# Two pairs of heads at once in the first layer of token mixing

## The chip, the cores and the metric

The kernel runs on one core of a Trainium2 chip. The metric is the device time in microseconds of one launch. The core's engines are TensorE (PE in the profile, with its weight loads as PEld), VectorE (DVE), ScalarE (ACT), GpSimd (POOL) and SyncE (SP, which issues the loads and stores). They run side by side and wait for each other through semaphores.

## The reference, cut to what matters

Everything is float32. There are 4 batches, 8 heads, 576 positions and a head width of 64, so `x` below is 4 x 576 x 512.

```
scores = q @ k.T / 8                          # per head, 576 x 576
keep   = scores >= rowmax(scores) - tau
attn   = exp(scores - rowmax) where keep, else 0
attn   = attn / (rowsum(attn) + 1e-9)
x      = attn @ v                             # heads side by side: 4 x 576 x 512

h = relu(x.T @ w_tok1) @ w_tok2               # token mixing: 576 -> 256 -> 576
u = x + h.T
y = u + relu(u @ w_ch1) @ w_ch2               # channel mixing: 512 -> 1536 -> 512

g = relu(y @ w_in)                            # 512 -> 1024
c = 3-tap convolution of g over positions
out = (g * sigmoid(c)) @ w_out                # 1024 -> 512
```

## The kernel before

**Split products.** Behind attention, each operand is split into a part rounded to the format fp32r ("h" in the name: `xh`, `wt1h`, `w1h`) and the rest (`xl`, `wt1l`, `w1l`), and a product is made of three matmuls: high by high, high by low, low by high. POOL makes the parts of `x` (`split_x`, L463), of the token weights (`split_wt`, L511), of the channel weights (`split_w1`, L472) and of the hidden tile (`split_hidden`, L482). A split is two instructions: a rounding copy and a subtraction.

**The attention loop.** The work runs over 16 pairs of heads, of one batch each time. A body `k` (g is the same number; inside the hardware loop over k = 4 to 13 it is a register) has five steps s = 0 to 4, one for each query tile of 128 (the last has 64 rows of both heads together). In body k, TensorE makes the scores two tiles ahead, the transposes of the masked probabilities of pair k, the product with v of pair k-1 (`times_v`, steps 0 and 1), and, for pair k-2, token mixing. The bodies go to k = 17. The chain of one tile is: TensorE's scores to PSUM; VectorE copies them out negated, with the row minimum (`copy_out`, L812); ScalarE takes the exponential (L585); VectorE masks and sums (`mask`, L829); TensorE transposes (L993); ScalarE drains (L597). The scores have one place in PSUM, so the next ones (`score_tails` and `scores`) wait for `max_done`, that is for `copy_out`.

**Each engine's order is written out by hand** in its `body`: TensorE's stands at L1136 and behind, ScalarE's at L685, VectorE's at L869, POOL's at L518, SP's below L395. An engine does its list in order, so a wait holds up all that is behind it.

**Token mixing of pair k-2 in body k.** At s=2 TensorE waits for `x_split` and makes the first layer (`mix_hidden`, L1058): for each of five token tiles (the last of 64 rows) and each of the three products one matmul, with the tile of x as the stationary operand (128 channels of the pair) and 256 weight columns moving, so 15 in all. Result: channels on partitions, 256 hidden units beside each other, in PSUM bank `mixed`. In front of them goes a transpose of the 64-row tail of x (L1068). ScalarE applies the relu (`drain_hidden`, L625) into `h1T`; at s=3 TensorE turns this by two transposes (`turn_hidden`, L1082), then turns the output of attention of pair k-1 (`turn_out`, L1045, and its tail, L1049). ScalarE drains the turned hidden tile to `h1f` (L633) behind its exponentials; POOL rounds it to `h1h` (L441) and subtracts to get `h1l` (L489). At s=4 TensorE turns x of pair k-1 (`turn_x`, L1055), waits for `tok_lo`, and makes the second layer (`mix_out`, L1095, 12 matmuls with 288 moving columns) into the banks `out_t` and `mixed`. ScalarE drains these (`drain_u`, L657) and POOL adds x (`add_u`, L496).

**Weights.** SP loads the token weights and the four parts of `w1` at the start. POOL splits the token weights in body 0 to 1 in three big pieces (L441, L455), as soon as the scores of pair 0 are done, and `w1` in 16 pieces of 384 columns (L448, L479), two in body 1, then one in each body to 15. All of w1 is waited for before the first matmul of channel mixing.

**The end of the loop.** Bodies 16 and 17 have no tiles of their own; between the rest of the mixing, TensorE makes the first four chunks of channel mixing's first layer (`hidden`, L1115): chunk 0 at s=3 and 1 at s=4 of body 16, 2 and 3 at s=2 and s=3 of body 17. They need `u` of batch 0 rounded (ScalarE, L684) and its rest (VectorE, L860). Behind the loop `project` (L1130) and `hidden` take turns; VectorE splits w2 between them.

The waits that the prediction speaks of, in the code:

```
def mix_out(pair, k):
    pe.wait_ge(tok_lo, pair + 1)
...
def split_wt():
    pool.wait_ge(s_done, NT)
...
if n == 0:
    pe.wait_ge(w1_split, PAIRS)
```

## Time and profile before

| | us |
|---|---|
| median of 3 runs | 893.38 (892.24 to 894.54) |
| the profiled execution, whole | 894.54 |
| its span in the trace | 892.7 |
| TensorE busy | 847.3 |
| VectorE busy | 429.5 |
| ScalarE busy | 411.2 |
| POOL busy | 278.4 |

The span is the time between the first and the last instruction of the trace. The profile's page gives each engine's busy time, the granted clock of TensorE in forty slices (in tenths of full speed), and the chain of work that ended last. "Waits" sum up which instruction waited for which. The chain of waits follows the work back from the last instruction, in order of time. The timeline lists single instructions with start and duration; matmuls are pipelined, so the duration of one is longer than the distance to the next. "Windows" gives each engine's busy time and the clock in stretches of time.

### The profile page before, as it was taken

Reading aid. Unit: us, or ns where it says so; the run is one execution under the profiler, and the core shown is the slowest. Engines: PE = TensorE matmul, PEld = TensorE weight load, DVE = VectorE, ACT = ScalarE, POOL = GpSimd, SP = SyncE. Lnnn points to the kernel's source line nnn. Section 1 sums busy time; section 2 is a strip of 40 time slices with the busy share of each in tenths; the row PEclk is TensorE's granted clock in tenths of the full one; section 3 lists DMA queues with packets and bytes.
Section 4 is the critical chain, followed back from the end, with each engine's and each line's share of the span. In section 5 each row is a group of like instructions: output and inputs, shape, how many; then the busy total and the mean of one; then the engine's idle time right before and its main releaser. Section 6 shows DMA issues by size and latency. Waiting matters only on the chain.

```text
span 892.7 us, 14832 instructions
## 1 busy us (share of the span) xinstructions
PE 847.3 (95%) x5544; PEld 665.0 (74%) x5544; DVE 429.5 (48%) x828; ACT 411.2 (46%) x866; POOL 278.4 (31%) x218
## 2 busy tenths in 40 slices
PE   7789989999999999889999999999999999999998
PEld 3456656666666666668888888888899989899996
DVE  5877767777777777271121121121121827437280
ACT  4577777777777777522111111121111737457371
POOL 0333333333333333252020020030075463618180
PEclk9799999999999999999999999999999999999999
DMA  9111111111111111400000000000040000010101
GB/s 270 51 50 47 49 48 48 47 47 47 47 47 47 47 48 16 142 1 1 1 1 0 1 1 1 0 1 1 5 161 25 2 23 26 1 59 0 47 0 59
DMA packets 20906, 33.75 MB, mean 38 GB/s; under 512 B 4416, under 2 KB 11136, under 8 KB 20864
## 3 DMA queue, kind: packets, MB, share of 16 engines
q1 hardware_dynamic: 20864, 33.18, 11.4%
q8 instruction: 28, 0.46, 0.2%
q14 instruction: 14, 0.11, 0.0%
HBM read 28.46 MB, written 4.72 MB: 37 GB/s over the span
## 4 chain that ended last, share of the span: by engine, by line
PE 88%; ACT 4%; issue 3%; DVE 2%; POOL 2%; ACTq 0%; POOLq 0%; DVEq 0%
PE score L1115 17%; PE score L1218 11%; PE score L974 6%; PE out_t L1130 4%; PE turn_y L1130 4%; PE mixed L1130 4%; PE tails L1130 4%; PE out_t L1030 4%; PE mixed L1073 4%; PE out_t L1203 4%; PE mixed L1030 4%; PE score L993 3%; PE turn_y L1203 2%; PE mixed L1203 2%; PE tails L1203 2%
## 5 line engine op out<-in xcount | busy, mean ns | idle before, releaser
L812 DVE TENSOR_SCALAR_CACHE_REDUCE negs<-score,neg_scale 128x576 f32<-128x576 f32 x144 | 112.7, 816 | 93.8 <-PE score L974 63.7
L890 DVE SCALAR_TENSOR_TENSOR h<-score,h 128x512 fp32r<-128x512 f32 (+1 forms) x60 | 38.3, 638 | 241.2 <-ACT h L677 241.2
L677 ACT ACTIVATE h<-score 128x512 fp32r<-128x512 f32 (+1 forms) x60 | 33.3, 555 | 255.3 <-PE score L1115 255.3
L829 DVE SCALAR_TENSOR_TENSOR prob<-negs,thresh,exps 128x576 f32<-128x576 f32 x144 | 140.6, 1009 | 0.3 <-ACT thresh L588 0.3
L585 ACT ACTIVATE exps<-negs,neg_max 128x576 f32<-128x576 f32 x144 | 104.9, 776 | 3.2 <-DVE negs L812 2.8
L1115 PE MATMUL score<-uh,w1h 128*128 128x512 f32 (+1 forms) x240 | 89.1, 371 | 3.2 <-DVE ul L860 3.2
L1115 PE MATMUL score<-uh,w1l 128*128 128x512 f32 (+1 forms) x240 | 89.0, 371 | 0.0
L1115 PE MATMUL score<-ul,w1h 128*128 128x512 f32 (+1 forms) x240 | 88.9, 370 | 0.0
L553 POOL TENSOR_TENSOR zl<-z,zh 128x512 fp32r<-128x512 f32 x32 | 54.8, 1711 | 98.7 <-ACT zh_t L751 98.7
L597 ACT ACTIVATE probT<-score 128x512 f32<-128x512 f32 x64 | 38.3, 598 | 80.2 <-PE turn_y L993 80.2
L974 PE MATMUL score<-qk 64*128 64x512 f32 x256 | 74.5, 659 | 0.0
L993 PEld LDWEIGHTS score<-ident,prob 64*128 64x128 f32 x512 | 41.8, 140 | 42.6 <-issue 42.1
L441 POOL TENSOR_SCALAR h1h<-h1f 128x256 fp32r<-128x256 f32 x16 | 7.4, 464 | 211.4 <-ACT h1f L633 211.4
L504 POOL TENSOR_TENSOR ul<-uy,uh 128x256 fp32r<-128x256 f32 (+6 forms) x7 | 16.7, 2398 | 173.9 <-ACT uh L664 173.9
L930 DVE SCALAR_TENSOR_TENSOR conv<-hpad,cw,conv 128x576 f32<-128x576 f32 x32 | 27.3, 853 | 77.5 <-ACT conv L764 77.5
L1218 PE MATMUL score<-yl,wih 128*128 128x288 f32 x256 | 54.8, 296 | 0.0
L1218 PE MATMUL score<-yh,wih 128*128 128x288 f32 x256 | 54.8, 296 | 0.0
L1218 PE MATMUL score<-yh,wil 128*128 128x288 f32 x256 | 54.8, 296 | 0.0
L1115 PEld LDWEIGHTS score<-uh,w1h 128*128 128x128 f32 x240 | 45.7, 190 | 11.3 <-issue 3.4
L1115 PEld LDWEIGHTS score<-ul,w1h 128*128 128x128 f32 x240 | 45.6, 190 | 7.7
L1115 PEld LDWEIGHTS score<-uh,w1l 128*128 128x128 f32 x240 | 45.6, 190 | 7.5
L940 DVE TENSOR_TENSOR z<-hpad,conv 128x576 f32<-128x576 f32 x32 | 50.5, 1578 | 1.1 <-POOL zl_t L555 1.1
(181 smaller groups left out, 2049.3 us busy)
## 6 DMA issues: line engine op xcount, KB each, us to landing
qk<-in_qk SPq DMA_DIRECT2D x16, 704.0 KB, 4.1
vm<-in_v SPq DMA_DIRECT2D x16, 320.0 KB, 4.3
result<-ostage SPq DMA_DIRECT2D x16, 256.0 KB, 2.1
w1f<-in_moe_w_ch SPq DMA_DIRECT2D x4, 768.0 KB, 10.7
w2f<-in_moe_w_ch SPq DMA_DIRECT2D x4, 768.0 KB, 7.0
wif<-in_moe_w_in SPq DMA_DIRECT2D x1, 2048.0 KB, 7.3
wof<-in_moe_w_out SPq DMA_DIRECT2D x8, 256.0 KB, 2.6
wt2f<-in_moe_w_tok SPq DMA_DIRECT2D x1, 576.0 KB, 10.0
```

What stands on the lines that cost most here:

```text
L553: nc.gpsimd.tensor_tensor(zl[:, t, :], z32[:, t % 2, 0:MAIN], zh[:, t, :].bitcast(F32), ALU.subtract)
L585: nc.scalar.activation(exps[i][:, h, :], negs[:, i, h, :], ACT.Exp, bias=neg_max[:, i, h:h + 1], scale=-1.0).then_inc(exp_done, 1)
L812: nc.vector.tensor_scalar(negs[:, i, h, :], raw_of[h], neg_scale[:, 0:1], None, ALU.mult, ALU.min, accum_out=neg_max[:, i, h:h + 1]).then_ ...
L829: nc.vector.scalar_tensor_tensor(out=prob[:, i, h * S:(h + 1) * S], in0=negs[:, i, h, :], scalar=thresh[:, i, h:h + 1], in1=exps[i][:, h, ...
L940: nc.vector.tensor_tensor(z32[:, t % 2, :], hpad[:, t % 3, 1:S + 1], conv[:, t % 3, :], ALU.mult) \
L974: mm = nc.tensor.matmul(score[:, 2 * h, :], qT[par][rows, t * P:(t + 1) * P], kT[par][rows, 0:MAIN])
L993: mm = nc.tensor.transpose(turn[r][:, to:to + D], prob[rows, i, k_at:k_at + P], ident[rows, rows])
L1030: nc.tensor.matmul(bank[mine, 0:HALF], vm[par][:, kt, mine], probT[par][:, h, kt, c * HALF:(c + 1) * HALF], start=(kt == 0), stop=False, s ...
L1115: mm = nc.tensor.matmul(hidden_banks[n % 4][:, 0:w], wt[:, c, kt, :], x[:, kt, 0:w], start=(kt == 0 and i == 0), stop=(kt == KM - 1 and i ...
L1130: mm = nc.tensor.matmul(sum_banks[mt][:, 0:w], wt[:, c, o:o + P], h3[:, n % RING, part, 0:w], start=(c == 0 and i == 0), stop=(c == KC - 1 ...
L1203: mm = nc.tensor.matmul(bank, z, wt[:, kt, :], start=(kt == 0 and n == 0), stop=(kt == KF - 1 and n == 2))
L1218: mm = nc.tensor.matmul(in_banks[c % 2][:, i, 0:HALF], wt[:, kt, c * P:(c + 1) * P], y[:, kt, i * HALF:(i + 1) * HALF], start=(n == 0), st ...
```

## The change

In the first layer a 128x128 tile of the weights becomes the stationary operand and x of two pairs (256 columns) the moving one. The result has hidden units on partitions, so the transposes of `turn_hidden` fall away, and `h1h`, `h1l`, `h1f`, `xh` and `xl` hold two pairs. ScalarE writes the rounded relu to `h1h` and once more in full to `h1f`; POOL only subtracts. `at.hid` is true for odd k from 3 on: both halves of the first layer (`i` = 0, 1: 128 hidden units each, both pairs k-3 and k-2), at s=2 and s=3. `at.mix` is true for even k from 4 on: the second layer of pair k-4 at s=2 and of pair k-3 at s=4. The bodies go to k = 18. The transpose of the 64-row tail of x goes to s=4, among the transposes of the probabilities. The 64-row weight tile is padded with zeros to 128 rows. `xh` and `xl` lie where the last five of twelve chunks of `w1h` come to lie, so these are split after the loop, and the other seven, of 512 columns, in bodies 1, 3, ..., 13. The token weights are split in seven pieces in bodies 1 and 2, once the scores of pair 1 are done.

```diff
--- before.py
+++ after.py
...
+            def split_x(at):
+                pair = at.g - 1
+                mine = slice((at.k - 1) % 2 * P, (at.k - 1) % 2 * P + P)
                 pool.wait_ge(x_done, pair + 1)
                 pool.wait_ge(short_x, pair + 1)
+                if at.hid:
+                    pool.wait_ge(tok_done, at.g - 1)
                 pool.nop(nofuse=True)
-                copy(xh[:, :, :], x32[:, :, :]).then_inc(xs_hi, 1)
+                copy(xh[:, :, mine], x32[:, :, :]).then_inc(xs_hi, 1)
                 pool.wait_ge(xs_hi, pair + 1)
                 pool.nop(nofuse=True)
-                nc.gpsimd.tensor_tensor(xl[:, :, :], x32[:, :, :], xh[:, :, :].bitcast(F32), ALU.subtract) \
+                nc.gpsimd.tensor_tensor(xl[:, :, mine], x32[:, :, :], xh[:, :, mine].bitcast(F32), ALU.subtract) \
                     .then_inc(x_split, 1)
...
+            def split_w1(c, wait):
+                if wait:
+                    pool.wait_ge(w1_loaded, KM * DMA)
                 pool.nop(nofuse=True)
...
+                hi, lo, f = (w[:, :, :, :].rearrange("p c k n -> p c (k n)") for w in (w1h, w1l, w1f))
+                copy_at(hi[:, c, :], f[:, c, :]).then_inc(chunk_hi, 1)
+                pool.wait_ge(chunk_hi, c + 1)
                 pool.nop(nofuse=True)
-                nc.gpsimd.tensor_tensor(lo[:, g, :], f[:, g, :], hi[:, g, :].bitcast(F32), ALU.subtract) \
+                nc.gpsimd.tensor_tensor(lo[:, c, :], f[:, c, :], hi[:, c, :].bitcast(F32), ALU.subtract) \
                     .then_inc(w1_split, 1)
...
-            def split_hidden(pair):
-                pool.wait_ge(hT_drained, pair + 1)
+            def rest_of_token(at, i):
+                pool.wait_ge(hid_left, at.g - 2 + i)
                 pool.nop(nofuse=True)
-                hi, lo = (h[:, :, :].rearrange("p t n -> p (t n)") for h in (h1h, h1l))
-                copy(hi, h1f[:, :]).then_inc(tok_hi, 1)
-                pool.wait_ge(tok_hi, pair + 1)
-                pool.nop(nofuse=True)
-                nc.gpsimd.tensor_tensor(lo, h1f[:, :], hi.bitcast(F32), ALU.subtract).then_inc(tok_lo, 1)
+                nc.gpsimd.tensor_tensor(h1l[:, i, :], h1f[:, i, :], h1h[:, i, :].bitcast(F32), ALU.subtract) \
+                    .then_inc(tok_lo, 1)
...
-            pool.wait_ge(set_once, 1)
-            def split_wt():
-                pool.wait_ge(s_done, NT)
+            pool.wait_ge(set_once, 2)
+            def split_wt(kts):
+                pool.wait_ge(s_done, 2 * NT)
                 pool.wait_ge(wt_loaded, 3 * DMA)
-                split_weight(wt1h[:, 0:FULL, :], wt1l[:, 0:FULL, :], wt1f[:, 0:FULL, :], wt_split)
-                split_weight(wt1h[0:TAIL, FULL, :], wt1l[0:TAIL, FULL, :], wt1f[0:TAIL, FULL, :], wt_split)
-                split_weight(wt2h[:, :, :], wt2l[:, :, :], wt2f[:, :, :], wt_split)
+                for kt in kts:
+                    split_weight(wt1h[:, kt, :], wt1l[:, kt, :], wt1f[:, kt, :], wt_split)
...
             def body(at):
-                g = at.g
-                if at.k == 1:
-                    split_wt()
+                g, k = at.g, at.k
                 if at.mix:
-                    split_hidden(g - 2)
+                    add_u(g - 4)
+                for i in range(KT if at.hid else 0):
+                    rest_of_token(at, i)
                 if at.pv:
-                    split_x(g - 1)
+                    split_x(at)
                 if at.mix:
-                    add_u(g - 2)
-                if at.k == 1:
-                    split_w1(0)
-                if at.units and at.k:
-                    split_w1(g)
+                    add_u(g - 3)
+                if k == 1:
+                    split_wt(range(NT))
+                if k == 2:
+                    for kt in range(KT):
+                        split_weight(wt2h[:, kt, :], wt2l[:, kt, :], wt2f[:, kt, :], wt_split)
+                if k % 2 == 1 and k < 2 * W1_EARLY:
+                    split_w1(g // 2, k == 1)
             bodies(pool, body)
+            for c in range(W1_EARLY, KC):
+                split_w1(c, False)
...
                     else:
+                        if r == 0 and at.pv:
+                            drain_x_tail(g - 1)
...
-            def drain_hidden(pair):
-                act.wait_ge(tok_done, pair + 1)
-                nc.scalar.activation(h1T[:, :], mixed[:, 0:DT], ACT.Relu).then_inc(relu_done, 1)
-                nc.scalar.activation(uy_pair[:, pair, MAIN:S], mixed[:, DT:DT + TAIL], ACT.Copy) \
-                    .then_inc(xt_tail_drained, 1)
-            def drain_turned(pair, k):
-                act.wait_ge(hT_done, pair + 1)
-                if k < PAIRS - 1:
-                    act.wait_ge(xa_tail_done, pair + 2)
-                nc.scalar.activation(h1f[:, :], mixed[:, 0:DT], ACT.Copy).then_inc(hT_drained, 1)
+            def drain_hidden(at, i):
+                act.wait_ge(tok_done, at.g - 2 + i)
+                nc.scalar.activation(h1h[:, i, :], mixed[:, 0:2 * P], ACT.Relu).then_inc(hid_hi, 1)
+                nc.scalar.activation(h1f[:, i, :], mixed[:, 0:2 * P], ACT.Relu).then_inc(hid_left, 1)
...
@@ -688,8 +694,6 @@
                 for s in range(NT):
                     if s == 2 and at.pv:
                         drain_out(g - 1, k - 1)
-                    if s == 2 and k == PAIRS:
-                        round_first_u(0)
...
@@ -697,24 +701,31 @@
                     ahead = at.unit(s + 2)
                     if ahead:
                         exp_unit(ahead)
-                    if s == 2 and at.mix:
-                        drain_hidden(g - 2)
-                    if s == 2 and k == PAIRS:
-                        round_first_u(1)
-                    if s == 2 and k == PAIRS + 1:
-                        unit(0, 2, 3)
-                    if s == 3:
+                    if s == 2:
                         if at.mix:
-                            drain_turned(g - 2, k - 2)
+                            drain_u(g - 4)
+                        if at.hid:
+                            drain_hidden(at, 0)
                         if at.pv:
                             normalise_short(g - 1, k - 1)
-                        if k >= PAIRS:
+                        if k == PAIRS:
+                            round_first_u(0)
+                            round_first_u(1)
+                        if k == PAIRS + 1:
+                            unit(0, 2, 3)
+                    if s == 3:
+                        if at.hid:
+                            drain_hidden(at, 1)
+                        if PAIRS <= k < PAIRS + 2:
                             unit(0, 3 * (k - PAIRS), 3 * (k - PAIRS) + 1)
                     if s == 4:
                         if at.pv:
+                            act.wait_ge(xt_done, g)
+                            if not at.units:
+                                drain_x_tail(g - 1)
                             drain_x(g - 1)
                         if at.mix:
-                            drain_u(g - 2, k - 2)
+                            drain_u(g - 3)
                         if k == PAIRS:
                             unit(0, 1, 2)
...
+            nc.vector.memset(wt1f[TAIL:P, FULL, :], 0.0).then_inc(set_once, 1)
...
-                    dve.wait_ge(tok_done, pair)
+                    dve.wait_ge(x_split, pair)
+                    dve.wait_ge(xt_done, pair)
...
+                    if at.pv:
+                        pe.wait_ge(short_x, g)
+                        pe.nop(nofuse=True)
+                        turn_x_tail()
...
-                    if k >= 2:
-                        pe.wait_ge(u_drained, 2 * (pair - 1))
+                    if k >= 4 and k % 2 == 0:
+                        pe.wait_ge(u_drained, 2 * (pair - 2))
+                    if k >= 3 and k % 2 == 1:
+                        pe.wait_ge(hid_left, pair - 1)
...
-            def turn_out(pair):
-                pe.wait_ge(out_drained, 2 * (pair + 1))
+            def turn_out(at):
+                if at.mix:
+                    pe.wait_ge(u_drained, 2 * (at.g - 4) + 1)
                 for t in range(FULL):
...
-            def mix_hidden(pair, k):
-                if k == 0:
-                    pe.wait_ge(wt_split, 3)
-                pe.wait_ge(x_split, pair + 1)
-                if k < PAIRS - 1:
-                    pe.wait_ge(out_drained, 2 * (pair + 2))
+            def mix_hidden(at, i):
+                g, k = at.g, at.k
+                if i == 0:
+                    if k == 3:
+                        pe.wait_ge(wt_split, NT + KT)
+                    pe.wait_ge(x_split, g - 1)
+                    if k > PAIRS:
+                        pe.wait_ge(u_drained, 2 * (g - 3))
                 else:
-                    pe.wait_ge(u_drained, 2 * pair)
-                pe.nop(nofuse=True)
-                nc.tensor.transpose(mixed[:, DT:DT + TAIL], x32[0:TAIL, FULL, :], ident[0:TAIL, 0:TAIL])
+                    pe.wait_ge(hid_left, g - 2)
+                    if at.pv:
+                        pe.wait_ge(short_x, g)
                 n = 0
                 for kt in range(NT):
-                    w = width[kt]
-                    for x, wt in ((xh, wt1h), (xh, wt1l), (xl, wt1h)):
-                        mm = nc.tensor.matmul(mixed[:, 0:DT], x[0:w, kt, :], wt[0:w, kt, :],
+                    for wt, x in ((wt1h, xh), (wt1l, xh), (wt1h, xl)):
+                        mm = nc.tensor.matmul(mixed[:, 0:2 * P], wt[:, kt, i * P:(i + 1) * P], x[:, kt, :],
                                               start=(n == 0), stop=(n == 3 * NT - 1))
                         n += 1
                 mm.then_inc(tok_done, 1)
...
-            def turn_hidden(pair):
-                pe.wait_ge(relu_done, pair + 1)
-                pe.wait_ge(xt_tail_drained, pair + 1)
-                for m in range(KT):
-                    mm = nc.tensor.transpose(mixed[:, m * P:(m + 1) * P], h1T[:, m * P:(m + 1) * P], ident[:, :])
-                mm.then_inc(hT_done, 1)
...
-            def mix_out(pair, k):
-                pe.wait_ge(tok_lo, pair + 1)
-                if k < PAIRS - 1:
-                    pe.wait_ge(x_done, pair + 2)
-                    pe.wait_ge(short_x, pair + 2)
+            def mix_out(at, i):
+                g, k = at.g, at.k
+                if i == 0:
+                    pe.wait_ge(tok_lo, g - 2)
+                    if k > PAIRS:
+                        pe.wait_ge(u_drained, 2 * (g - 4))
+                else:
+                    pe.wait_ge(u_drained, 2 * (g - 3))
+                    if at.pv:
+                        pe.wait_ge(x_done, g)
+                        pe.wait_ge(short_x, g)
                 for c, bank in enumerate((out_t, mixed)):
                     n = 0
                     for kt in range(KT):
                         for h, wt in ((h1h, wt2h), (h1h, wt2l), (h1l, wt2h)):
-                            mm = nc.tensor.matmul(bank[:, 0:HALF], h[:, kt, :], wt[:, kt, c * HALF:(c + 1) * HALF],
+                            mm = nc.tensor.matmul(bank[:, 0:HALF], h[:, kt, i * P:(i + 1) * P],
+                                                  wt[:, kt, c * HALF:(c + 1) * HALF],
                                                   start=(n == 0), stop=(n == 3 * KT - 1))
                             n += 1
                     mm.then_inc(u_done, 1)
...
-                    pe.wait_ge(w1_split, PAIRS)
...
+                if m == 0:
+                    pe.wait_ge(w1_split, c + 1)
...
-                    if at.mix and s == 2:
-                        mix_hidden(g - 2, k - 2)
+                    if s == 2:
+                        if at.pv:
+                            turn_out_tail(g - 1)
+                        if at.hid:
+                            mix_hidden(at, 0)
+                        if at.mix:
+                            mix_out(at, 0)
                         if k == PAIRS + 1:
                             hidden(2)
                     if s == 3:
-                        if at.mix:
-                            turn_hidden(g - 2)
                         if at.pv:
-                            turn_out(g - 1)
-                            turn_out_tail(g - 1)
-                        if k >= PAIRS:
+                            turn_out(at)
+                        if at.hid:
+                            mix_hidden(at, 1)
+                        if PAIRS <= k < PAIRS + 2:
                             hidden(3 * (k - PAIRS))
                     if at.pv and s == 4:
+                        if not at.units:
+                            pe.wait_ge(short_x, g)
+                            pe.nop(nofuse=True)
+                            turn_x_tail()
                         turn_x(g - 1, k - 1)
                     if at.mix and s == 4:
-                        mix_out(g - 2, k - 2)
+                        mix_out(at, 1)
                         if k == PAIRS:
                             hidden(1)
```

## Rows read from the trace of the kernel before

**Rows 1.** The page: busy time of the engines, and granted clock in forty slices.
```profile
PE 847.3 (95%) x5544; PEld 665.0 (74%) x5544; DVE 429.5 (48%) x828; ACT 411.2 (46%) x866; POOL 278.4 (31%) x218
...
PEclk9799999999999999999999999999999999999999
```

**Rows 2.** Waits, 0 to 400 us: total us, times, longest.
```profile
PE out_t L1095 <- POOL h1l L489: 18.4, 14, 2.2
```

**Rows 3.** The chain of waits through bodies 7 and 8: start, duration, what.
```profile
160.28 1.06 PE score L974 x4
...
166.81 1.06 PE out_t L1095 x6
...
168.89 1.06 PE score L974 x4
...
173.01 1.06 PE score L974 x4
...
180.34 2.16 PE mixed L1073 x15
...
182.91 1.06 PE score L974 x4
```

**Rows 4.** Timeline, steps 3 and 4 of the same body: start, duration, instruction.
```profile
161.92 0.38 PE L1082 MATMUL mixed<-ident,h1T 128*128 128x128 f32 x2
162.14 0.60 PE L1045 MATMUL out_t<-ident,oT 128*128 128x128 f32 x4
...
164.79 0.66 PE L1055 MATMUL tails<-ident,x 128*128 128x128 f32 x4
...
164.84 0.39 ACT L633 ACTIVATE h1f<-mixed 128x256 f32<-128x256 f32 x1
```

**Rows 5.** Masks and POOL: the masks' line (min/median/max ns), then the timeline.
```profile
L829 DVE SCALAR_TENSOR_TENSOR prob<-negs,thresh,exps x144: 754/817/2893, 13.1 to 362.7; 128x576 f32<-128x576 f32 x144
...
166.20 1.16 DVE L829 SCALAR_TENSOR_TENSOR prob<-negs,thresh,exps 128x576 f32<-128x576 f32 x1
...
172.67 1.54 DVE L829 SCALAR_TENSOR_TENSOR prob<-negs,thresh,exps 128x576 f32<-128x576 f32 x1
...
172.27 1.32 POOL L479 TENSOR_TENSOR w1l<-w1f,w1h  x1 [0.15 <-POOL w1h L448]
```

**Rows 6.** Timeline of body 0: the row sum, and a split on POOL.
```profile
28.72 2.47 DVE L837 TENSOR_SCALAR rowsum_pos<-rowsum 128x9 f32<-128x9 f32 x1
...
22.54 2.73 POOL L455 TENSOR_TENSOR wt1l<-wt1f,wt1h 128x1024 fp32r<-128x1024 f32 x1
```

**Rows 7.** Bodies 0 to 3: timeline, the chain, a window (clock is the third last).
```profile
22.74 1.13 PE L974 MATMUL score<-qk 64*128 64x512 f32 x4
...
50.99 1.08 PE score L974 x4
...
54.23 1.13 PE L974 MATMUL score<-qk 64*128 64x512 f32 x4
...
54.48 2.09 DVE L829 SCALAR_TENSOR_TENSOR prob<-negs,thresh,exps 128x576 f32<-128x576 f32 x1
...
77.85 1.13 PE L974 MATMUL score<-qk 64*128 64x512 f32 x4
...
30.00:32.00 2.00, 0.02 (x2) 0.00 (x0) 2.00 (x4) 0.97 (x4) 1.16 (x1) 0.50 0.01 4
```

**Rows 8.** The end of the loop: chain, then a window (clock third last).
```profile
374.87 0.96 issue
...
383.11 4.58 PE score L1115 x12
...
403.06 0.97 PE out_t L1130 x3
...
414.23 2.72 PE score L1115 x12
...
384.00:388.00 4.00, 4.00 (x15) 3.14 (x15) 2.53 (x2) 0.27 (x1) 3.83 (x2) 0.63 0.01 4
```

More of the change, by code:

```diff
@@ L91, in build @@
     w1f = nc.alloc_sbuf_tensor_at("w1f", [P, KC, KM, P], F32, offset=w1l_at)
-    w1_pieces = [w[:, :, :, :].rearrange("p c k n -> p (c k n)").rearrange("p (g n) -> p g n", g=PAIRS)
-                 for w in (w1h, w1l, w1f)]
+    W1_EARLY = 7
+    x_parts = Region(w1l_at - 2 * size([P, NT, 2 * P]))
+    xh = x_parts.put("xh", [P, NT, 2 * P], F32R)
+    xl = x_parts.put("xl", [P, NT, 2 * P], F32R)
+    assert x_parts.at == w1l_at and w1l_at - 2 * size([P, NT, 2 * P]) >= fixed.at + W1_EARLY * size([P, KM, P])
     w2l_at = ch1.at
@@ L133, in build @@
     x32 = s1.put("x32", [P, NT, P])
-    xh = s1.put("xh", [P, NT, P], F32R)
-    xl = s1.put("xl", [P, NT, P], F32R)
-    h1T = s1.put("h1T", [P, DT])
-    h1f = s1.put("h1f", [P, DT])
+    h1f = s1.put("h1f", [P, KT, 2 * P])
     u_part = s1.put("u_part", [P, S])
-    h1h = s1.put("h1h", [P, KT, P], F32R)
-    h1l = s1.put("h1l", [P, KT, P], F32R)
+    h1h = s1.put("h1h", [P, KT, 2 * P], F32R)
+    h1l = s1.put("h1l", [P, KT, 2 * P], F32R)
     wt1h = s1.put("wt1h", [P, NT, DT], F32R)
@@ L310, in __init__ @@
                 self.pv = 1 <= k <= PAIRS
-                self.mix = k >= 2
+                self.hid = k % 2 == 1 and 3 <= k
+                self.mix = k % 2 == 0 and 4 <= k
             def unit(self, n):
@@ L333, in bodies @@
                     body(Pair(2 * j + par, FIRST + par))
-            for k in range(LAST, PAIRS + 2):
+            for k in range(LAST, PAIRS + 3):
                 body(Pair(k, k))
@@ L357, in build @@
         EARLY = 4
+        SHORT_AT = BANK - P
         block = ctx.enter_context(nc.Block())
@@ L639, in normalise_short @@
                 if k >= 1:
-                    act.wait_ge(tok_done, pair)
+                    act.wait_ge(x_split, pair)
                 for h in range(2):
@@ L648, in drain_x, with drain_u @@
             def drain_x(pair):
-                act.wait_ge(xt_done, pair + 1)
                 nc.scalar.activation(uy_pair[:, pair, 0:MAIN], tails[:, :], ACT.Copy).then_inc(xt_drained, 1)
-            def drain_u(pair, k):
+            def drain_u(pair):
                 for c, bank in enumerate((out_t, mixed)):
                     act.wait_ge(u_done, 2 * pair + c + 1)
-                    if c == 0 and k >= 1:
+                    if c == 0 and not (isinstance(pair, int) and pair == 0):
                         act.wait_ge(u_added, pair)
@@ L977, in scores, with turn_x_tail @@
                 mm.then_inc(s_done, 1)
+            def turn_x_tail():
+                return nc.tensor.transpose(turn[0][:, NT * D:NT * D + TAIL], x32[0:TAIL, FULL, :], ident[0:TAIL, 0:TAIL])
             def turn_probs(at, t):
@@ L1048, in turn_out_tail @@
             def turn_out_tail(pair):
-                nc.tensor.transpose(mixed[:, DT:DT + P], oT[:, MAIN:MAIN + 2 * TAIL], ident[:, :]).then_inc(xa_tail_done, 1)
+                pe.wait_ge(out_drained, 2 * (pair + 1))
+                nc.tensor.transpose(mixed[:, SHORT_AT:BANK], oT[:, MAIN:MAIN + 2 * TAIL], ident[:, :]).then_inc(xa_tail_done, 1)
             def turn_x(pair, k):
```

17 lines of the change are left out of this document (6 added, 11 removed).

## The prediction

> **What bounds the kernel now.** The page came first. TensorE is busy for 95% of the span (VectorE for 48%), and its granted clock is full but for a dip in the second of forty slices, 22 to 45 us [rows 1]. So only two things can pay: less work on TensorE, or less time in which it stands still. The attention loop ends near 400 us of 892.7; nothing that the change touches acts behind it, except where the last five chunks of w1 are split.
>
> The waits of the first 400 us say who keeps TensorE standing: of the waits that stand before a matmul the largest entry is POOL's h1l, 18.4 us in 14 [rows 2]. The chain of waits through one pair shows its place [rows 3]. From scores to scores a pair takes 182.91 - 160.28 = 22.63 us. Each of its five steps begins with its scores: s=3 with s=4 take 8.61 us (to 168.89), s=0 4.12 (to 173.01), s=1 with s=2 9.90. In s=4 the second layer of token mixing stands at the end of a row of engines: ScalarE drains the turned hidden tile at 164.84, behind its exponentials, POOL rounds it and subtracts, and TensorE starts at 166.81, having ended turn_x at 165.45: 1.36 us of nothing [rows 3, 4]. 14 x 1.36 = 19 us, the 18.4 of the waits.
>
> Then what stands right behind, since it is late next. VectorE's copy of the scores, which has to be out before the next ones are written, is a floor: in k=1, with no mixing at all, one step still takes 54.23 - 50.99 = 3.2 us [rows 7]. And VectorE's masks take 0.82 us in the median but 1.16 and more, up to 1.54, while POOL computes [rows 5]: the two of s=4, from 166.20, end near 168.6, when TensorE, late itself, has not begun the scores of 168.89. This is hidden today by the 1.36 us.
>
> **The change part by part.**
>
> *Matmuls of the first layer: nothing.* Each instruction now has a weight tile as stationary and two pairs (256 columns) as moving operand; before it had the x tile and 256 weight columns. Two pairs took 2 x 15 instructions of 256 columns and take 2 x 15 now, each with its own load. 15 of them take 2.16 us [rows 3]; before and behind the last three of 64 rows some 0.1 us is lost each, and those are now padded to 128 rows: -0.2 us a pair.
>
> *Turning the hidden tile: gone.* The two transposes L1082 and their switch lie between 161.92 and 162.14 [rows 4]: -0.22 us a pair. ScalarE has two relus of 128x256 (0.39 each by L633 [rows 4]) in place of relu and copy: nothing. POOL loses the rounding h1h, less than half of the 1.6 us from 165.23 to 166.81 [rows 3, 4]. The x tail's transpose only moves from s=2 to s=4; turn_out_tail moves from s=3 to s=2: nothing.
>
> *The order.* Odd k carries both first layers (s=2, s=3), even k both second layers (s=2, s=4), each of pairs whose hidden tile was ready one k earlier. The 1.36 us wait goes. What comes in its place, in us after the scores of s=3 (160.28):
> Odd k: turned probabilities (L1045 ends them, in 0.44 [rows 4]) and turn_out end near 2.1, 15 matmuls with their switch to 4.2, next scores at 4.6 (now 3.14). The new wait for hid_left is covered: both relus follow the matmuls of s=2, which end 0.5 before, so they are done at 0.3, and TensorE asks at 2.1. In s=4 only turn_x is left, so the copy is the floor: scores 4.6 to 5.65, copy done at 7.2, next scores 7.6. s=3 and s=4 take 7.6 us against 8.61: -1.0. VectorE starts the masks of the next tile at 7.3. POOL, which takes the two subtractions, xh, xl and then a w1 chunk, works until about 12.4, so these masks are long, 2.4 us together as those from 166.20 on [rows 5], and end at 9.7. TensorE has its scores at 8.65 and wants them: +1.0 in s=0 of the even k.
> Even k: s=3 has only turn_out and sits on the floor, 3.14. s=4: scores to 4.2, turning to 5.3, mix_out 1.86 to 7.2, next scores 7.4: -1.2 against 8.61. Masks end at 8.2 even if long, before TensorE's 8.5. ScalarE drains u until 8.95, and times_v asks for it at 8.9: +0.1. mix_out in s=2 is 1.86 where 2.16 and the tail's bubble were: -0.25. s=1 loses its wait for long masks, since POOL has nothing but add_u there: -0.3 in both kinds.
> Sum for odd and even: (-1.0 - 0.2 - 0.3 + 0.1) + (-1.2 + 1.0 - 0.25 - 0.3) = -2.15 us in two pairs, -1.1 a pair. For k=3 to 15 that is 13 x 1.1 = -14.3 us. Bounds: without any long mask on the path -1.65 a pair (-21.5); if two thirds of it are taken back, -0.5 a pair (-6.5). I take -1.1, because the long masks are in the rows of every pair.
> At this place the Trainium skill speaks against the change (SBUF - State Buffer, "Who interferes with whom"): a VectorE instruction with two SBUF inputs waits for a GpSimd instruction that reads SBUF to end, and the other way round. The trace agrees: a sum of 9 numbers took 2.47 us while wt2l ran [rows 6]. By that rule each POOL instruction can add at most its own length, and w1 pieces grow from 384 to 512 columns. What it would make if it decides is rival C.
>
> *Splitting the token weights: later and in small pieces.* Now they are split in k=0. The longest mask of all, 2.89 us [rows 5], stands beside wt1l (from 22.54 on), a row sum of 9 columns takes 2.47 us beside wt2l; TensorE starves, and from 30 us on the clock is at 1.2 GHz, for some ten us [rows 6, 7]. After the change the pool waits for the scores of k=1 and takes 256 or 576 columns at a time. k=0 and k=1 then go by undisturbed steps: from scores at 22.74, s=3 and s=4 3.1 (the floor, without turn_x), s=0 4.1, s=1 5.0, s=2 2.6 (one head to copy), s=3 and s=4 3.3 each, which is 47.2 for the scores of k=2's s=0, now 54.23 [rows 3, 7]: -7.0 us. The splits then fall on k=2, whose first two masks already take long (2.09 us) beside two w1 pieces [rows 7], and on the first step of k=3: +0.7, by half a long pair of masks. Bounds of this part: 0 (the same stall and dip elsewhere) to -10.
>
> *Work that moves to the end.* k=2 mixes nothing. Now k=2 takes 54.23 to 77.85 = 23.6 us; without mixing 5.5 + 5.2 + 2.6 + 3.3 + 3.2 = 19.8: -3.9 us, which must come back. The end now: from the last times_v (374.87) to the first project (403.06) 28.2 us [rows 8]. New, counted from T, the same point: mix_out of pair 12 to T+2.9, turn_out 3.45; then the rounding of u on ScalarE and its rest on VectorE, the same four instructions as now, one place later for ScalarE and with fewer in front of them, and so hidden(0) at T+8.0, as now (383.11, which is 8.24); with a clock dip as now (0.63 [rows 8]), 4.4 us; turn_x and mix_out 13 to 14.7, hidden(1) 17.5, first layer 19.5, hidden(2) 22.2, first layer 24.1, hidden(3) 26.9, mix_out 14 to 28.6, mix_out 15 (waits 0.5 for the drain) 30.9, drained 31.45, project at T+31.5: +3.3 us. Bounds +1 and +8 (5 more of clock, by the ten half-speed us of k=0).
> The five late w1 chunks take POOL about 3 us each, of it 1.32 x 4/3 for the subtraction by the 384-column piece [rows 5], from about T+33; so the one that hidden(7) needs is there at T+36. Now hidden(5) begins 11.2 us behind the first project [rows 8], hidden(7) thus 22 behind, at T+53: nothing. If that cover were gone, 3 us. The added xh/xl wait (tok_done) stands in front of the POOL queue of add_u and w1 only, both with many us of room. SP's queue issues the same loads at the same places. The zeroing of 64x256 is one short instruction before the first scores' copy: nothing, at most 0.3.
>
> **The sum.** -7.0 + 0.7 - 3.9 - 14.3 + 3.3 = -21.2 us. The profiled execution took 894.54 us (span 892.7), which gives 873.3; it was the slowest of the three, 1.2 above the median 893.38, so the forecast is 872.2, rounded 872 us.
>
> **The rivals.**
> *A, the loop keeps the whole gap*: POOL's shorter work frees the masks, -1.65 a pair, 872 - 7 = 865 us. For: POOL loses the rounding and a third of w1. Against: its work in the odd k stays in one piece from 5.4 to 12.4. Chance 0.14.
> *B, the start gives nothing*: the token splits stall k=1 to k=3 as they did k=0, or the clock dips there. 872 + 7 = 879, with a dip at the end as well 883. For: the same engines, and 54.48's mask already took 2.09 us [rows 7]. Against: pieces of 0.7 to 1.4 us, and TensorE has turning and times_v there. Chance 0.2.
> *C, slower*: VectorE becomes the bound. If the masks of s=4 and s=0 take 2.09 us each (as at 54.48) and not 1.2, those of s=4 end 1.8 us later, TensorE waits that in each k, and the copy queued behind them pushes s=1 by some 0.6: +2.4 a pair, 13 x 2.4 = +31, 903 us. It decides from 1.85 us a pair (24 us) on. For: the copies, masks and sums are all on VectorE, and nothing behind them moves without them. Against: VectorE has a quarter of each pair to spare, and a mask as long came up once after k=0 [rows 5, 7]. Chance 0.08.
> *D, the end*: clock at half for ten us more in k=16 to k=18, 877. Chance 0.08.
>
> **How the numbers follow.** The forecast has 0.5, with a range of its own of 866 to 879. With A at 865 and B and D inside, 861 to 885 holds a bit over 0.8; C and part of B's upper end lie outside. About 0.3% (2.7 us) is what can be told from no change. Faster: forecast, A, D and nearly all of B, 0.88; same 0.04 (between B's end and C); slower 0.08.
>
> **What would show it.** The wait of TensorE for h1l is gone, and no wait for hid_left or tok_lo over 0.5 us stands in its place. Odd and even k alternate, near 21.2 and 21.9 us. Scores of k=2 begin near 47 us with a clock of 1.0 throughout; no mask over 2.2 us in the first 50 us. From the last times_v to project 31 to 32 us. It is wrong if masks of about 2 us stand in every pair, if the clock dips again before 60 us, or if the stretch from project on changes its length by over 1 us.

## The result, and the profile after

The changed kernel takes 868.71 us in the median of 4 runs (868.62 to 869.71); the kernel before, run beside it, 893.86. The ratio is 0.9724, with a 95% interval of 0.9707 to 0.9741: faster by 2.8%, or 24.7 us. The forecast was 872 us, with a range of 861 to 885.

The page of the kernel after, the lines that answer to [rows 1]:

```profile
PE 826.0 (95%) x5512; PEld 655.8 (76%) x5512; DVE 420.9 (49%) x829; ACT 411.0 (47%) x866; POOL 263.7 (30%) x202
...
PEclk9999999999999999899999999999999999999999
```

The dip of the clock in the second slice is gone; in the seventeenth one shows, which was shorter before (there the clock was 0.63 from 384 to 388 us [rows 8]). Its waits over the first 400 us, the three in front of TensorE's matmuls that matter, in total us, times, longest (compare [rows 2]):

```profile
PE score L975 <- DVE negs L824: 15.6, 22, 1.5
...
PE score L1010 <- DVE prob L841: 7.7, 8, 1.1
...
PE score L1142 <- DVE ul L873: 6.1, 1, 6.1
```

The 18.4 us for POOL's h1l are gone from the loop. In their place other waits have grown: for VectorE's copies of the scores from 9.8 us to 15.6, for its masks (L841, as L829 before) from 3.1 to 7.7, and one at the end from 3.2 to 6.1. The chain of waits through bodies 7 and 8 (compare [rows 3]; L987 and L989 are the scores, L1099 the first layer, L1120 the second):

```profile
156.00 1.06 PE score L987 x4
...
161.04 0.92 PE score L989 x2
...
162.96 1.79 PE mixed L1099 x15
164.75 0.22 PE score L975 x2
164.97 1.06 PE score L987 x4
...
167.22 1.79 PE mixed L1099 x15
...
169.24 1.08 PE score L987 x4
...
172.04 2.72 DVE prob L841 x4
...
178.00 1.06 PE score L987 x4
...
183.04 0.91 PE score L989 x2
...
186.77 1.06 PE score L987 x4
...
198.22 1.06 PE score L987 x4
```

From scores of s=1 to the next such scores the odd body takes 178.00 - 156.00 = 22.0 us, the even one 198.22 - 178.00 = 20.2 us, together 42.2 where two bodies took 45.3. The lines left out of this chain are TensorE's, the copies of the scores, and ScalarE's exponentials and drains at the end of the even body, behind which TensorE stands for 0.18 us. Its longest wait in these bodies is for the masks from 172.04 on, at the turn from the odd to the even body: 1.11 us. The timeline shows what lies beside them (start, duration, instruction; in brackets how long the engine stood before it):

```profile
172.05 2.07 POOL L472 TENSOR_TENSOR xl<-x,xh 128x640 fp32r<-128x640 f32 x1
...
172.64 2.10 DVE L841 SCALAR_TENSOR_TENSOR prob<-negs,thresh,exps 128x576 f32<-128x576 f32 x1
...
174.89 0.25 PE L1010 MATMUL score<-ident,prob 64*128 64x64 f32 x1 [1.11 <-DVE prob L841]
```

At the start, the first scores of body 2 come at 47.04, not 54.23 [rows 7], and those of body 3 at 65.92, not 77.85:

```profile
47.04 1.13 PE L987 MATMUL score<-qk 64*128 64x512 f32 x4
...
65.92 1.13 PE L987 MATMUL score<-qk 64*128 64x512 f32 x4
```

The end of the loop (compare [rows 8]), the chain of waits and one window, whose third last number is the clock:

```profile
346.94 0.39 issue
...
350.56 2.56 DVE ul L873
353.37 4.88 PE score L1142 x12
...
369.75 0.39 ACT h1h L639
370.55 1.99 POOL h1l L491
372.58 1.06 PE out_t L1120 x6
...
377.33 0.95 PE out_t L1157 x3
...
353.00:357.00 4.00, 3.63 (x9) 2.89 (x10) 2.74 (x3) 0.00 (x0) 0.00 (x0) 0.50 0.00 0
```

Between 346.9 and 353.4 TensorE has nothing but waits for the rest of the first chunk of u, and `hidden(0)` (L1142) then runs mostly at 1.2 GHz. From the last times_v (344.0) to the first project (377.33) it is 33.3 us, 28.2 before. From there to the end both kernels need the same: 867.0 - 377.33 = 489.7 and 892.7 - 403.06 = 489.6.

The account of the two spans, cut by the scores (forecast behind the stroke): to body 2 -7.2 us / -7.0, body 2 -4.7 / -3.9, body 3 to the last times_v -18.9 / -13.6, from there to project +5.1 / +3.3; together -25.7, the difference of the spans, / -21.2.

### The profile page after: what moved, and what is told of

Its sections match the earlier page's. It is cut to its first block, busy times and chain, and to the rows that moved or that the text cites. A ratio compares the mean times of both kernels' runs of the same rounds, so it can differ in the third digit from the quotient of the medians.

```text
span 867.0 us, 14725 instructions
## 1 busy us (share of the span) xinstructions
PE 826.0 (95%) x5512; PEld 655.8 (76%) x5512; DVE 420.9 (49%) x829; ACT 411.0 (47%) x866; POOL 263.7 (30%) x202
## 4 chain that ended last, share of the span: by engine, by line
PE 86%; DVE 5%; ACT 4%; issue 4%; DMA 1%; POOL 0%; DVEq 0%; ACTq 0%; SPq 0%; POOLq 0%
PE score L1142 17%; PE score L1253 12%; PE score L987 5%; PE out_t L1157 4%; PE turn_y L1157 4%; PE mixed L1157 4%; PE tails L1157 4%; PE out_t L1053 4%; PE out_t L1238 4%; PE mixed L1053 4%; PE mixed L1099 3%; PE score L1010 3%; PE turn_y L1238 3%; PE mixed L1238 3%; PE tails L1238 3%
## 5 line engine op out<-in xcount | busy, mean ns | idle before, releaser
L683 ACT ACTIVATE h<-score 128x512 fp32r<-128x512 f32 (+1 forms) x60 | 33.3, 555 | 256.5 <-PE score L1142 256.5
L841 DVE SCALAR_TENSOR_TENSOR prob<-negs,thresh,exps 128x576 f32<-128x576 f32 x144 | 133.7, 960 | 0.3 <-ACT thresh L595 0.3
L1142 PE MATMUL score<-uh,w1h 128*128 128x512 f32 (+1 forms) x240 | 89.2, 372 | 6.1 <-DVE ul L873 6.1
L1142 PE MATMUL score<-ul,w1h 128*128 128x512 f32 (+1 forms) x240 | 89.0, 371 | 0.0
L1142 PE MATMUL score<-uh,w1l 128*128 128x512 f32 (+1 forms) x240 | 89.0, 371 | 0.0
L1010 PEld LDWEIGHTS score<-ident,prob 64*128 64x128 f32 x512 | 41.0, 139 | 45.3 <-issue 45.2
L987 PE MATMUL score<-qk 64*128 64x512 f32 x256 | 72.3, 641 | 0.0
L1142 PEld LDWEIGHTS score<-uh,w1h 128*128 128x128 f32 x240 | 45.8, 191 | 13.9 <-issue 6.3
L499 POOL TENSOR_TENSOR uy<-u_part,uy 128x576 f32 (+1 forms) x16 | 23.5, 1471 | 96.9 <-ACT u_part L663 96.9
L1010 PE MATMUL score<-ident,prob 64*128 64x64 f32 x512 | 44.6, 224 | 7.8 <-DVE prob L841 7.7
L1142 PEld LDWEIGHTS score<-uh,w1l 128*128 128x128 f32 x240 | 45.7, 190 | 7.7
L1142 PEld LDWEIGHTS score<-ul,w1h 128*128 128x128 f32 x240 | 45.7, 190 | 7.6
```

Source lines behind the costliest of these rows:

```text
L841: nc.vector.scalar_tensor_tensor(out=prob[:, i, h * S:(h + 1) * S], in0=negs[:, i, h, :], scalar=thresh[:, i, h:h + 1], in1=exps[i][:, h, ...
L987: mm = nc.tensor.matmul(score[:, 2 * h, :], qT[par][rows, t * P:(t + 1) * P], kT[par][rows, 0:MAIN])
L1010: mm = nc.tensor.transpose(turn[r][:, to:to + D], prob[rows, i, k_at:k_at + P], ident[rows, rows])
L1142: mm = nc.tensor.matmul(hidden_banks[n % 4][:, 0:w], wt[:, c, kt, :], x[:, kt, 0:w], start=(kt == 0 and i == 0), stop=(kt == KM - 1 and i ...
```

## The experiments

Ratios are to the kernel before, run on the same chip in turns, with 95% intervals.

### The token weights later, alone (e1)

```diff
 def split_wt():
-    pool.wait_ge(s_done, NT)
+    pool.wait_ge(s_done, 2 * NT)
-    split_weight(wt1h[:, 0:FULL, :], ...)
+    for kt in range(FULL):
+        split_weight(wt1h[:, kt, :], ...)
...
-    split_weight(wt2h[:, :, :], ...)
+    for kt in range(KT):
+        split_weight(wt2h[:, kt, :], ...)
```

It is called behind `split_x` in body 1.

> The kernel before, with one part of the change alone: the token weights are split in seven pieces of 256 and 576 columns once the scores of pair 1 are done, in body 1, not in three big ones once those of pair 0 are. Theory (the stall of body 0 and the clock's fall behind it are made by these splits and don't come back): scores of body 2 near 49 us in place of 55.3, the clock full throughout the first 50 us, 886 to 888 us in all. Rival (the stall only moves to bodies 1 and 2, or the clock falls there): 892 or more.

890.82 us, ratio 0.9961 (0.9947 to 0.9976): between the two. Scores of body 2 begin at 47.71, so the stall of body 0 is gone and didn't come back in body 1. But in this kernel body 2 mixes already, and its first layer waits 2.50 us for the last piece. The chain of waits of this kernel:

```profile
60.67 1.78 POOL wt2l L455
62.46 0.14 issue
62.59 0.24 PE mixed L1069
62.84 3.65 PE mixed L1074 x15
```

15 matmuls take 3.65 us in place of 2.16: behind the wait the clock is at half for 3.4 us, from 62.9 on. From scores to scores, s=2 of body 2 takes 8.72 us, not 4.70. The seven runs lie between 888.6 and 892.9 us, the shorter ones with the higher mean clock; only one of the longer was traced. The late moment thus pays only where body 2 doesn't mix, as in the change.

### The token weights at the early moment, in small pieces (e8)

```diff
 def split_wt():
     pool.wait_ge(s_done, NT)
-    split_weight(wt1h[:, 0:FULL, :], ...)
+    for kt in range(FULL):
+        split_weight(wt1h[:, kt, :], ...)
...
-    split_weight(wt2h[:, :, :], ...)
+    for kt in range(KT):
+        split_weight(wt2h[:, kt, :], ...)
```

> The kernel before, with the token weights split at the early time of body 0, but in seven small pieces. Theory by size (a long POOL subtraction blocks one mask for its whole length): no mask over 1.6 us, body 1 begins 2 us earlier or more, and with TensorE less idle the clock stays full, 887 to 889. Rival by moment (POOL is busy at body 0 in any case and blocks mask behind mask): the same stall, clock dip near 29 us, 892 to 895.

888.35 us, ratio 0.9938 (0.9923 to 0.9953): the theory by size. Beside pieces of 256 columns the two masks that took 0.94 and 2.89 us now take (its timeline):

```profile
22.18 1.12 DVE L831 SCALAR_TENSOR_TENSOR prob<-negs,thresh,exps 128x576 f32<-128x576 f32 x1
...
22.65 0.91 POOL L441 TENSOR_SCALAR wt1h<-wt1f 128x256 fp32r<-128x256 f32 x1
...
23.23 0.94 DVE L831 SCALAR_TENSOR_TENSOR prob<-negs,thresh,exps 128x576 f32<-128x576 f32 x1
```

The clock stays full until 377 us. One expectation failed, that no mask takes over 1.6 us: one of 1.95 stands beside the second layer's piece of 576 columns, and one of 2.08 (at 49.41) beside `xl`.

```profile
29.51 1.79 POOL L455 TENSOR_TENSOR wt2l<-wt2f,wt2h 128x576 fp32r<-128x576 f32 x1
...
29.97 1.95 DVE L831 SCALAR_TENSOR_TENSOR prob<-negs,thresh,exps 128x576 f32<-128x576 f32 x1
```

The scores of body 2 begin at 49.16, where they began at 54.23 before and begin at 47.04 in the change. So the size of the pieces is the greater part of the start's gain, 5.1 us here and 5.5 in all; the moment is the smaller.

### Distance alone (e2), and with small pieces (e10)

The kernel before, one pair at a time with its transposes, but `mix_out`, `drain_u` and `add_u` for pair k-3, and `h1h` and `h1l` in two buffers each:

```diff
-    h1h = s1.put("h1h", [P, KT, P], F32R)
+    h1h = [s1.put(f"h1h{i}", [P, KT, P], F32R) for i in range(2)]
...
-                    if at.mix and s == 4:
-                        mix_out(g - 2, k - 2)
+                    if at.out and s == 4:
+                        mix_out(g - 3, k - 3)
```

> The kernel before, with one pair at a time as it was, transposes and all, but the second layer of token mixing one body later (pair k-3, hidden tile in two buffers). Theory (the loop's gain is the wait for POOL's h1l, which distance alone removes): bodies of 21.4 us in place of 22.6, 13 of them, some 3 us back at the end, 880 to 884 us. Rival (the gain comes from two pairs at once: no transposes, no ScalarE copy, other matmul forms): bodies of 22.2 or more, 889 or more.

881.81 us, ratio 0.9871 (0.9856 to 0.9886). Bodies 3 to 14 take 21.7 us each, copy to copy, where they took 22.6. The clock's dip at the start is still there. So distance alone is worth 11.5 us, 0.9 us a body.

e10 adds the diff of e8 to this one.

> The kernel before with two parts at once: the second layer one body later, and the token weights in seven small pieces at the early time. What is left to the changed kernel is two pairs at once with weights stationary, no transposes of the hidden tile, the padded tile. If the parts add: 893.8 - 12 - 5.4 = 876.4 us, and the new form of the first layer is worth some 7.5 us (868.7). If the form is worth nothing: 869 to 871.

877.74 us beside 894.69, ratio 0.9811 (0.9796 to 0.9826), which is -16.9 us on 893.8; e2 and e8 by themselves give -11.5 and -5.5, so these parts add. The change has -24.7. The rest, 7.8 us (the two intervals leave 6 to 10), belongs to what e10 lacks: two pairs at once, no transposes, the padded tile, the later moment and the split of w1.

### The last tile at 64 rows again (e3, e9)

```diff
+                    w = width[kt]
...
-                        mm = nc.tensor.matmul(mixed[:, 0:2 * P], wt[:, kt, i * P:(i + 1) * P], x[:, kt, :],
+                        mm = nc.tensor.matmul(mixed[:, 0:2 * P], wt[0:w, kt, i * P:(i + 1) * P], x[0:w, kt, :],
```

> The changed kernel, with the last token tile of the first layer at 64 rows again (its matmuls read half of the rows; the sums are the same). Theory (TensorE loses time at each change between 64 and 128 rows): 15 matmuls of the first layer take 2.0 to 2.2 us in place of 1.79, 16 times, 872 to 874 us. Rival (the height costs nothing, the first layer's steps became shorter for another reason): 1.8 us, 868.7.

882.78 us, ratio 0.9874 (0.9859 to 0.9889): 14 us slower than the change, three times what the theory said. The height costs what was said: in each odd body s=2 and s=3 are 0.39 and 0.37 us longer. The rest is in the chain, TensorE's waits and a window of this kernel in the turn from body 5 to body 6:

```profile
133.80 3.31 DVE prob L841 x4
...
137.86 1.16 PE out_t L1053 x4
...
135.74 0.24 PE L1010 MATMUL score<-ident,prob 64*128 64x64 f32 x1 [0.39 <-DVE prob L841]
...
137.25 0.24 PE L1010 MATMUL score<-ident,prob 64*128 64x64 f32 x1 [1.05 <-DVE prob L841]
...
137.00:141.00 4.00, 3.75 (x22) 2.12 (x24) 3.15 (x10) 2.59 (x5) 1.22 (x1) 0.57 0.00 0
```

Two masks hold the chain for 3.31 us, not 2.72, TensorE stands twice (1.44 us in all, where it stood 1.06 us in the change), and the clock falls for 3.4 us. Of the six turns of the loop four have the fall and take 7.6 to 7.8 us for s=0; two, with the same waits (0.43 and 1.04 us at 181), have none and take 6.1 to 6.2, where the change takes 5.5 to 5.6. To tell height from this, e9 puts the same edit on e7 (below), in which POOL leaves these masks alone.

> The last token tile of the first layer at 64 rows again, this time in the kernel whose POOL leaves the masks alone (x split first, w1 behind the masks; 862.9 us with 128 rows). Theory (of the 14 us that 64 rows cost in the changed kernel some 5.5 are TensorE's changes of height, 0.39 + 0.37 us in each of 7 odd bodies; the rest is that the masks came to lie worse beside POOL's reads, and the clock fell in the wait behind them): no dip in the loop, 867.5 to 869.5 us. Rival (the height itself costs all of it): 875 to 877.

867.16 us against 862.89 with 128 rows: 4.3 us for the height by the medians, 3.6 by the ratios (0.9695 and 0.9655), a little less than said, and no dip in the loop. The chain of e9, 15 matmuls and the scores' first piece behind them, to be compared with 162.96 and 164.75 above:

```profile
162.11 1.97 PE mixed L1104 x15
164.08 0.42 PE score L979 x2
```

1.97 for 1.79 and 0.42 for 0.22: 0.19 us on each of two changes of height.

### POOL's order in odd bodies (e4, e7)

```diff
-                for i in range(KT if at.hid else 0):
-                    rest_of_token(at, i)
+                if at.hid:
+                    rest_of_token(at, 0)
                 if at.pv:
                     split_x(at)
+                if at.hid:
+                    rest_of_token(at, 1)
```

> The changed kernel, with one POOL order changed in odd bodies: the split of x goes ahead of the second subtraction of the hidden tile, so that it begins some 1.5 us earlier and ends near where the masks of the next pair's first tile begin. Theory (that mask takes 2.10 us because it waits for POOL's 2.07 us subtraction of x, and TensorE waits for the mask): the mask takes 1.3 us or less, odd bodies get 0.5 to 1.0 us shorter, 7 of them, 862 to 865 us. Rival (POOL then has the w1 chunk beside the same mask, which blocks it as long): no change, 868 to 869.

867.77 us, ratio 0.971 (0.9696 to 0.9723): the rival, near enough; the turn takes 5.3 us and not 5.5. The split of x is over before the masks, but the w1 chunk now lies beside them (timeline of e4):

```profile
171.84 1.56 POOL L448 TENSOR_TENSOR w1h<-w1f,ones 128x512 f32 x1
...
172.43 1.58 DVE L843 SCALAR_TENSOR_TENSOR prob<-negs,thresh,exps 128x576 f32<-128x576 f32 x1
```

e7 takes this chunk away as well:

```diff
+                if k % 2 == 0 and 4 <= k <= 2 * W1_EARLY:
+                    pool.wait_ge(mask_done, TILES * g + 4)
+                    split_w1(g // 2 - 1, False)
...
-                if k % 2 == 1 and k < 2 * W1_EARLY:
-                    split_w1(g // 2, k == 1)
```

(chunk 0 stays in body 1.)

> The changed kernel with the split of x ahead of the second subtraction, and the w1 chunk of an odd body taken in the next even body, behind the masks of its second tile. Theory (in odd bodies TensorE waits for two masks, and they for whatever POOL reads then; with nothing beside them they take 0.82 us): the masks at the turn from odd to even bodies take 0.8 to 1.1 us, odd bodies 21.2 us or less in place of 22.2, 861 to 864 us. Rival (VectorE's own queue is the floor there): 867 to 868.

862.89 us, ratio 0.9655 (0.9642 to 0.9668). By its chain of waits the odd body takes 174.72 - 153.73 = 21.0 us, 22.0 in the change:

```profile
153.73 1.06 PE score L991 x4
...
174.72 1.06 PE score L991 x4
```

The two masks of the turn (timeline of e7):

```profile
169.69 1.03 DVE L845 SCALAR_TENSOR_TENSOR prob<-negs,thresh,exps 128x576 f32<-128x576 f32 x1
...
170.65 0.81 DVE L845 SCALAR_TENSOR_TENSOR prob<-negs,thresh,exps 128x576 f32<-128x576 f32 x1
```

So what POOL does beside the masks costs the change 1.0 us at each of the six turns from an odd body to an even one, 5.8 us in all.

### The end (e5), and all together (e6)

```diff
+                    if s == 0 and k == PAIRS:
+                        round_first_u(0)
+                        round_first_u(1)
...
+                    if s == 3 and at.k == PAIRS:
+                        dve.wait_ge(pv_done, PAIRS)
+                        split_first_u()
```

The first is ScalarE's, the second VectorE's, ahead of `normalise`; the same calls are taken out of their old places.

> The changed kernel, with the first chunk of u rounded on ScalarE in step 0 of body 16, where it stands idle, and its rest taken by VectorE as soon as the last times_v is done, ahead of POOL's split of x. Theory (at the end the matmuls of hidden(0) wait 6 us for that rest, which is behind ScalarE's list and blocked by POOL, and the clock then halves for 6.8 us): the wait falls under 1 us and the dip goes, 860 to 863 us. Rival (TensorE has nothing else, the time only moves to the first mix_out or to w2): 867 or more.

861.11 us, ratio 0.9632 (0.9619 to 0.9645). The chain of e5 has `hidden(0)` right behind `turn_out`, at full clock:

```profile
346.94 0.44 PE out_t L1070 x4
347.38 2.76 PE score L1143 x12
```

e6 is e5 and e7 in one.

> The changed kernel with early rounding of u, the split of x ahead of the second subtraction of the hidden tile, and the w1 chunks behind the masks in even bodies. If the three gains add: 855 to 859 us. If the later w1 chunks only block other masks: the same as with early rounding alone, less 1 us.

854.67 us, ratio 0.956 (0.9547 to 0.9573), 14 us under the changed kernel: the gains of e5 (7.6) and e7 (5.8) add. It is the fastest version here.

## Why the prediction was right, point by point

The forecast was 3.5 us above the measured median, and 4.5 us short in the two traces. That is what is left of errors that went both ways: the loop gained 5.3 us more than forecast, the start 1.0 more, and the end cost 1.8 more.

**The wait for h1l.** Right, mechanism and place. e2 shows it without the rest of the change. The forecast of -1.1 us a body came out as -1.5 (45.3 to 42.2 for two), while distance alone brings 0.9. Counted as the prediction does, from s=0 to s=0, in us between the scores (the measured ones by the timeline, bodies 9 and 8):

| | before | odd k, forecast | odd k | even k, forecast | even k |
|---|---|---|---|---|---|
| s=0 | 4.12 | 4.2 | 4.43 | 5.1 | 5.52 |
| s=1 and s=2 | 9.90 | 9.4 | 8.97 | 9.35 | 8.77 |
| s=3 and s=4 | 8.61 | 7.6 | 7.51 | 7.4 | 7.02 |
| body | 22.6 | 21.2 | 20.9 | 21.9 | 21.3 |

**The step s=2: mis-sized.** This is the term with the largest error: 1.0 us too little gain in two bodies, more than the whole gap of 0.9. From scores to scores, s=2 took 4.59 us; forecast were 4.4 (odd) and 4.35 (even), measured 161.04 to 164.97, 3.93, and 183.04 to 186.77, 3.73. In the odd body the fault is in "15 of them take 2.16 us ... -0.2 us a pair". I charged two changes of height inside the 15 matmuls at 0.1 each. There were four in this step: into L1068, a transpose of 64 rows, out of it, into the last three matmuls, and out of them, the last of which shows only in the scores' first piece (0.42 for 0.22). e9 measures two of these at 0.19 each. That L1068's two cost the same is argued from this, not shown by a run. The Trainium skill says (TensorEngine Tiling (Array Packing), section Key Properties) that changing the tiling mode drains the engine. The runs agree in sign and give a price, 0.19 us; that these matmuls do change the mode no run shows. In the even body there is a second fault: the second layer was taken at 1.86 us, its time behind a wait (1.06 and 0.80 [rows 3]). With no wait in front of it, it takes 0.79 and 0.80.

**The masks beside POOL.** The mechanism is right, and the masks end 9.8 us after the scores of s=3, where 9.7 was said; s=0 of the even body grew by 1.4 us, not 1.0. Of this e7 gives back 1.0. Only the instructions were off by a place: xl begins at 172.05 and lies beside both masks, and the second takes 2.10 us, rather than both 1.2 each. e4 shows that a piece of w1 in that place does it as well (1.58 us); in e7, with nothing of POOL's beside it, the second takes 0.81. The rule of the Trainium skill that the prediction cites (SBUF - State Buffer, "Who interferes with whom") agrees with these masks. The sum of 9 numbers [rows 6], given there as its example, is none: it has one input.

**Rival A** had nearly the right size for the loop (-1.65 us a body, measured -1.5), but its mechanism didn't come: the long masks stay on the path, 1.1 us at each turn, and what was gained beyond the forecast came from s=2.

**Rival C** didn't come, but e3 shows that it was not far: 0.4 us more in two steps moved the masks so that they took 3.3 us in place of 2.7, the clock fell behind the wait in four of six turns, and 4.3 us of height became 14.

**The start.** Forecast 47.2 for body 2's scores, measured 47.04. Some luck is in this: s=3 of body 0 began 0.6 us earlier than before, which scatters from run to run (21.84 to 22.80 in the kernels here); from there it is 24.9 us, 24.5 by the forecast. Body 2 without mixing took 18.9 where 19.8 was said. That the size of the pieces counts more than the moment (e8 against e1) the prediction had left open. Rival B didn't come, but the +0.7 that was charged did: s=0 and s=1 of body 3 take 5.04 and 5.22 us, where body 9 takes 4.43 and 4.95, 0.9 us more. TensorE stands for a mask beside `xl` and a piece of the token weights, and the next mask takes 1.95 us beside another:

```profile
67.99 0.24 PE L1010 MATMUL score<-ident,prob 64*128 64x64 f32 x1 [0.70 <-DVE prob L841]
...
70.28 1.95 DVE L841 SCALAR_TENSOR_TENSOR prob<-negs,thresh,exps 128x576 f32<-128x576 f32 x1
```

**Work at the end.** Forecast +3.3, measured +5.1. All of the 1.8 us is `hidden(0)`. It began at T+9.3 rather than T+8.0: ScalarE rounds u behind `normalise_short`, and VectorE's rests, beside POOL's xl, take 4.04 us where they took 2.55. And its dip of the clock is 6.8 us long where it was 3.4, so it takes 4.88 and not 4.4. The dip is rival D in a small form. In the last body POOL's h1l takes 1.99 us beside VectorE's subtraction of w2, not 0.73, and stands in the chain above; but it costs next to nothing, since TensorE is busy with `hidden(3)` until 372.46 and begins mix_out of pair 14 at 372.58.

**What was costed at nothing.** The late w1 chunks are hidden: from project on, both kernels take the same 489.6 us. The waits for hid_left and tok_done don't appear in the loop.

## What to carry to other kernels

Where a short product of several engines stands in front of the bounding one, put the consumer one turn of the loop later before making the product cheaper: here distance alone gave nearly half of the gain. Count the changes between short and full tiles on TensorE (those of transposes, as far as argued here, too), and pad the last tile where zeros are free. Then look at which two-input instructions of VectorE have a POOL instruction beside them at the moment that TensorE waits for them: cutting one-time splits into small pieces was worth 5.5 us (e8), moving POOL's work away from two masks 5.8 (e7), and ordering the one-time work at the loop's end 7.6 (e5).

## What the runs showed of the hardware

A wait of TensorE costs more than its length where the granted clock falls behind it. In e3 TensorE stood 0.4 us longer at a turn than in the changed kernel, 1.44 us in two pieces, and in four of six turns the clock was at 1.2 GHz for some 3.4 us behind this. At the other two the waits were as long and the clock stayed full; what tells them apart is open. In the changed kernel, with one wait of 1.1 us a turn, it didn't fall in the loop. At 1.2 GHz the four groups of times_v took 3.6 us in place of 2.1.

A VectorE instruction on 9 columns and a mask of 576 are held alike until the POOL instruction beside them ends: the first ended at 31.19 us and wt2l at 31.16; the mask of 2.89 us ended at 25.89 and wt1l at 25.27. This delay is the same everywhere: in the traces of before and after, every one of the 73 masks over 1.15 us ended 0.60 to 0.62 us behind the end of a POOL instruction that began before it, be it h1l, xh, xl, a piece of w1 or add_u. The 189 masks with no POOL instruction beside them took 0.75 to 0.82 us. It goes the other way too: xl took 2.07 us where a mask was running when it began (172.05), and 1.54 at 45.65 with none.
